# Two feed-forward layers: GpSimd's long subtractions in pieces, early stores moved ahead, one addition moved up

## The reference, cut to what matters

```
g = x @ w_gate;  val = x @ w_val
x = ((g * sigmoid(g)) * val) @ w_out            # first network, hidden width 1536
h = x @ w_in
g = where(h >= 1, h, where(h <= -1, 0, (h + 1)**2 / 4))
out = g @ w_out2                                # second network, hidden width 2048
```

## Time and profile before

| what | value |
|---|---|
| median of 3 runs | 982.42 us (982.23 to 983.0) |
| the profiled execution's own time | 983.68 us |
| its span | 981.9 us |
| TensorE busy | 967.0 us |
| VectorE, ScalarE, GpSimd busy | 704.1, 463.7, 305.1 us |
| chain that ended last: TensorE's share | 86% |

### The profile page before, as it was taken

How to read it: one execution, slowest core, us unless ns; L and a number is a source line. 1 busy time by engine, 2 the same in 40 slices (tenths; PEclk the granted TensorE clock), 3 DMA queues, 4 the chain that set the end, 5 groups by cost and what they waited for, 6 DMA issues and landing times.

```text
span 981.9 us, 18870 instructions
## 1 busy us (share of the span) xinstructions
PE 967.0 (98%) x6372; PEld 926.6 (94%) x6372; DVE 704.1 (72%) x1369; ACT 463.7 (47%) x940; POOL 305.1 (31%) x291
## 2 busy tenths in 40 slices
PE   8999999999999999999999999999999999999998
PEld 7777777999999999999999999999999999999998
DVE  6888989577777555557555568888886777867766
ACT  6899999655445223234222336544543334433331
POOL 5777776166672000100001156575310010000000
PEclk9999999999999999999999999999999999999999
DMA  7554543389878655555555534767775744538321
GB/s 247 166 160 150 170 146 106 122 302 339 321 268 333 244 193 208 223 222 214 217 194 193 207 124 179 251 232 274 277 262 194 286 170 184 208 147 298 138 106 65
DMA packets 46156, 204.72 MB, mean 209 GB/s; under 512 B 5488, under 2 KB 5872, under 8 KB 46064
## 3 DMA queue, kind: packets, MB, share of 16 engines
q1 hardware_dynamic: 45920, 203.52, 56.9%
q10 hardware_dynamic: 144, 0.00, 0.0%
HBM read 147.33 MB, written 56.17 MB: 207 GB/s over the span
## 4 chain that ended last, share of the span: by engine, by line
PE 86%; ACT 5%; issue 3%; DVE 3%; DMA 2%; POOL 1%; SPq 0%; ACTq 0%; DVEq 0%; POOLq 0%
PE ps L1454 25%; PE ps L1455 24%; PE ps L1456 24%; PE ps L1425 5%; PE ps L1368 5%; ACT pt L809 3%; PE ps L1398 3%; DMA kept_ul<-wu_l 1%; DVE xt_l L1109 1%; ACT tmp L919 0%; PE ps L1344 0%; DMA wu_r<-w_up 0%; DVE xy L1224 0%; ACT xt_h L840 0%; DVE negs L1048 0%
## 5 line engine op out<-in xcount | busy, mean ns | idle before, releaser
L1454 PE MATMUL ps<-xt_h,wu_h 128*128 128x384 f32 x840 | 281.4, 335 | 2.7 <-ACT u2s L889 1.7
L1456 PE MATMUL ps<-xt_h,wu_l 128*128 128x384 f32 x840 | 280.8, 334 | 0.0
L1455 PE MATMUL ps<-xt_l,wu_h 128*128 128x384 f32 x840 | 280.8, 334 | 0.0
L1454 PE MATMUL ps<-hid_h,wd_h 128*128 128x384 f32 x672 | 225.5, 336 | 2.9 <-DVE xy L1224 2.4
L1455 PE MATMUL ps<-hid_l,wd_h 128*128 128x384 f32 x672 | 224.6, 334 | 0.0
L1456 PE MATMUL ps<-hid_h,wd_l 128*128 128x384 f32 x672 | 224.6, 334 | 0.0
L1224 DVE TENSOR_TENSOR xy<-xy,ps 128x384 f32<-128x384 f32 x288 | 158.6, 551 | 69.9 <-PE ps L1456 69.1
L904 ACT ACTIVATE hid_h<-hid_r 128x768 fp32r<-128x768 f32 x84 | 70.7, 842 | 201.7 <-DVE hid_r L1198 139.7
L1454 PEld LDWEIGHTS ps<-xt_h,wu_h 128*128 128x128 f32 x840 | 157.7, 188 | 4.6 <-issue 3.5
L1455 PEld LDWEIGHTS ps<-xt_l,wu_h 128*128 128x128 f32 x840 | 157.7, 188 | 0.0
L1456 PEld LDWEIGHTS ps<-xt_h,wu_l 128*128 128x128 f32 x840 | 157.7, 188 | 0.0
(11 more groups left out here) (87 smaller groups left out, 1282.4 us busy)
## 6 DMA issues: line engine op xcount, KB each, us to landing
wu_l<-kept_ul SPq DMA_DIRECT2D x40, 896.0 KB, 7.5
wu_h<-kept_uh SPq DMA_DIRECT2D x40, 896.0 KB, 5.2
kept_uh<-wu_h SPq DMA_DIRECT2D x20, 896.0 KB, 6.8
kept_ul<-wu_l SPq DMA_DIRECT2D x20, 896.0 KB, 8.5
wd_h<-kept_dh SPq DMA_DIRECT2D x28, 512.0 KB, 3.7
wd_l<-kept_dl SPq DMA_DIRECT2D x28, 512.0 KB, 4.7
wu_r<-w_up SPq DMA_DIRECT2D x20, 512.0 KB, 5.1
qk<-qk_in SPq DMA_DIRECT2D x15, 640.0 KB, 4.9
```

The lines of the kernel that those rows point to most:

```text
L1454: nc.tensor.matmul(dst, w_hi, v_hi, start=start, stop=False, skip_group_check=onto)
L1455: nc.tensor.matmul(dst, w_hi, v_lo, start=False, stop=False, skip_group_check=onto)
L1456: return nc.tensor.matmul(dst, w_lo, v_hi, start=False, stop=stop, skip_group_check=onto)
```

## The change

Four edits. **(1)** `up_low` and `down_low` and `x_sum` on GpSimd are issued in pieces: 768 columns as 3 of 256, 512 columns as 2 of 256, and an activation sum of 768 as 2 of 384; the semaphore is raised by the last piece. **(2)** The stores of steps 0 and 1 (three of the four) are issued right after `read_r` of the last pair, ahead of `load_down(0)`; the low part of step 1 follows in step 0. **(3)** In later steps the store of the high part stands ahead of `load_up(u + 2)` and the store of the low part behind it, as before. **(4)** On VectorE, in steps 37 to 43, the first addition `add_down(units[0])` stands ahead of `g_half(u - 1, 1)` instead of behind it.

```diff
-            def keep_up(u):
+            def keep_up_high(u):
                 n = step_index(u)
                 for k in range(3):
                     sp.wait_ge(wu_hi[k], computed_before(u) + 1)
                 sp.dma_start(kept_uh[n].rearrange("p (k n) -> p k n", k=7), wu_h[u % 2][:].bitcast(F32)).then_inc(up_kept_h[u % 2], 16)
+
+            def keep_up_low(u):
+                n = step_index(u)
                 for k in range(3):
                     sp.wait_ge(*low_count(u, k))
                 sp.dma_start(kept_ul[n].rearrange("p (k n) -> p k n", k=7), wu_l[u % 3][:, 1:8].bitcast(F32)).then_inc(up_kept_l[u % 3], 16)
...
             read_r(NPAIR - 1)
+
+            keep_up_high(0)
+            keep_up_low(0)
+            keep_up_high(1)
             for u in range(STEPS):
...
+                if u > 1 and computed(u):
+                    keep_up_high(u)
                 if 0 < u and u + 2 < STEPS:
                     load_up(u + 2)
-                if computed(u):
-                    keep_up(u)
+                if u > 1 and computed(u):
+                    keep_up_low(u)
+                if u == 0:
+                    keep_up_low(1)
...
-                nc.gpsimd.tensor_tensor(wu_l[u % 3][:, a:b], wu_r[u % 3][:, a:b], wu_h[u % 2][:, a - 1:b - 1].bitcast(F32),
-                                        ALU.subtract).then_inc(low_pool[n], 1)
+                for k in range(a, b):
+                    low = nc.gpsimd.tensor_tensor(wu_l[u % 3][:, k], wu_r[u % 3][:, k], wu_h[u % 2][:, k - 1].bitcast(F32),
+                                                  ALU.subtract)
+                low.then_inc(low_pool[n], 1)
...
-                nc.gpsimd.tensor_tensor(wd_l[:, t % 6], wd_r[:, t % 6], wd_h[:, t % 6].bitcast(F32),
-                                        ALU.subtract).then_inc(wd_lo, 1)
+                for a in (0, DM // 2):
+                    cols = slice(a, a + DM // 2)
+                    low = nc.gpsimd.tensor_tensor(wd_l[:, t % 6, cols], wd_r[:, t % 6, cols],
+                                                  wd_h[:, t % 6, cols].bitcast(F32), ALU.subtract)
+                low.then_inc(wd_lo, 1)
...
-                nc.gpsimd.tensor_tensor(raw_sum(sb, n), a, b, ALU.subtract).then_inc(tp, 1)
+                for k in range(2):
+                    part = nc.gpsimd.tensor_tensor(raw_sum(sb, n)[:, k], a[:, k], b[:, k], ALU.subtract)
+                part.then_inc(tp, 1)
...
                 if u > STEPS1:
                     hid_low(tiles_of(u)[0] - 2)
+                    if computed(u):
+                        add_down(units[0])
                     g_half(u - 1, 1)
-                add_down(units[0])
+                if u == STEPS1 or not computed(u):
+                    add_down(units[0])
```

## The result

The changed kernel takes 979.44 us (median of 8 runs, 979.08 to 980.37) where the kernel before takes 982.73 (8 runs): ratio 0.9966, 95% interval 0.9957 to 0.9976, so 2.4 to 4.2 us less. The profiled execution took 979.51 us with a span of 977.7. Forecast were 979.3 and a gain of 3.1.

The account below looks back on a forecast made before the run. TensorE, busy 967.0 of 981.9 us, was taken as the bound. From 983.68 with the profiler, 1.8 for the stores and 1.3 for the second network gave 980.6; the median, 1.26 below, 979.3; range 975.2 to 983.2.

Parts of the forecast that it names:

- The ceiling: TensorE's eight feed-forward waits, 5.4 us listed, each cost about 0.26 more: at most 7.5 us to win.
- The early stores: Around 204 us, stores issued before 184.5 let load_up(3) go earlier and end the u2s wait: 1.8 us gained.
- with sums from 198.9 it just does: Start of step 3: VectorE's up_low(3, 0), after the four sums, ends by 203.5, in time for product 0.
- Pieces in the first network: GpSimd's instructions get longer there by cutting, but TensorE waits for none of this.
- Turns: Second network's step starts: VectorE and GpSimd exclude each other and alternate by instruction; that network gains 1.3 us in sum.
- The walk: Turn-by-turn count of VectorE's chain at step starts: 0.98 us waiting at 41 and 42; 0.58, 0.68 and 0.2 at 38.
- Steps 40 to 42: Start of step 40 loses 0.1 us, starts of 41 and 42 gain 1.4, within step 42 another 0.8.
- The moved addition: VectorE, second network: the first addition ahead of g_half comes early but puts g_half 0.47 us later in the chain.
- (a): Rival: all eight TensorE waits go, 975.4 us; chance 0.20 for a gain of 5 to 8.
- (b): Rival: pieces do nothing on balance or the second network gives back the stores' gain, 982.1 us; 0.25 together with (d).
- (c): Rival: g_half behind the addition lengthens VectorE's chain, needing 1.5 us waiting a start; slower, 986 us; chance 0.10.
- (d): Rival: the early stores do not help, since the load lands late, 981.5 us; chance 0.25 together with (b).

Follow-up runs that it names:

- e9_second_whole: e5_second with GpSimd's down_low of tiles 0, 36 and 37 whole again, one instruction of 512 columns each; 977.04 us, ratio 0.9938 to the kernel before.
- e1_stores: The kernel before with only the store edits 2 and 3, GpSimd's instructions whole and the additions in their old order; 982.42 us, ratio 0.9995.
- e3_move: The kernel before with only edit 4, the first addition moved ahead of g_half; 983.61 us, ratio 1.001.
- e10_early_only: e1_stores with the high part of later steps again stored behind load_up, so edit 2 alone; 982.21 us, 1 run.
- e5_second: The changed kernel with the second addition, add_down(units[1]), also moved ahead of the second hid_low in steps 37 to 43; 977.82 us, ratio 0.9950.
- e4_no_move: The changed kernel with the first addition back in its old place, so edits 1 to 3; 980.38 us, ratio 0.9978 to the kernel before.
- e12_behind: The changed kernel with both additions between g_half and the second hid_low; 982.11 us, ratio 0.9989 to the kernel before.
- e11_order_only: e1_stores with both additions moved ahead and every GpSimd instruction whole, no pieces; 979.01 us, ratio 0.9958 to the kernel before.
- e7_fine: The changed kernel with the weights' low parts in pieces of 128 columns instead of 256; 982.02 us, ratio 0.9989 to the kernel before.

## Why the prediction came out right, point by point

**The ceiling.** That a wait costs 0.26 more than listed, 7.5 us in all, held: e9_second_whole removes all but one of the eight and its span is 6.7 us shorter, 6.4 of it in the feed-forward part; its time is 6.1 less.

**The early stores.** The mechanism was right at each step (stores at 183 to 184, load near 191, first sum at 198.9), the size was not: 1.3 instead of 1.8. A wait at the start of step 3 for `up_low` was one of the prediction's own signs of being wrong, and it came (0.25 listed). The term that failed is "with sums from 198.9 it just does". The four sums took 4.0 us, not 3, because VectorE's operations took turns with them, and VectorE's own `up_low(3, 0)` then waited for a piece. e1_stores shows the same wait longer, with a whole instruction in place of the piece. The 1.8 was also counted from a single execution, whose wait for `u2s` was 1.65; in the unchanged code of e3_move it was 1.06, and from there only 0.6 is gained. By the medians the stores gave 0.4 alone and 1.1 beside the pieces. That edit 3 is worth nothing rests on the one execution of e10_early_only.

**Pieces in the first network** cost TensorE nothing: between product (2, 6) and step 36 the lag changes by 0.1 us in all.

**Turns.** The claim that an instruction of GpSimd stands before each operation of VectorE's chain, and that the sums slip into it, is what the rows at 614 us show: a sum before `s_half` and one before `hid_low`. The starts of 37 and 38 gave back time, at the down that waits for the second addition, as forecast; e5_second, which changes only that addition's place, removes both waits. At step 37 I had 1.1 us lost and it was 0.5. The walk has 0.58 + 0.68 + 0.2 = 1.46 us of turns at step 38, and step 37 "behaves alike". Over an unhindered 0.95, VectorE's three operations wait 0.36 + 0.54 + 0.07 = 0.97 at step 38 and 0.31 + 0.54 + 0.07 = 0.92 at step 37, where `s_half` takes 1.26, `hid_low` 1.49 and `g_half` 1.02. That is 0.2 more than in the kernel before, so with the 0.47 of the moved addition the second one comes 0.7 us later and not 1.1. One of the signs named did not come as stated: the sums began 0.8 us later in their steps, not 0.3 to 0.6 (at 657.79 against 658.37, with a lag of -1.4).

**Steps 40 to 42.** Here the walk was too dark. It had 0.98 us of turns before the second addition, the rows show 0.57, and the half microsecond of slack holds it but for 0.05. So the forecast waits at 41 and 42 did not come, and step 40 gained 0.6 instead of losing 0.1. This is 1.1 us in the trace, and with the 0.6 of step 37 it outweighs the 0.5 of the stores: the trace is 1.3 us better than the sum. The median is 3.3 us lower and the span 4.2, because the profiled execution of the kernel before was 0.9 us slower than its median; 0.6 of that is the longer wait at 204 us. The other profiled executions began the feed-forward part 0.3 us earlier to 0.7 later than that one. That 979.44 lies so close to the forecast of 979.3 is luck in part: the stores gave less and the second network more than forecast, and both sizes were counted from one execution.

**The moved addition.** I priced it as a cost of 0.47 in the chain. e3_move bears that out at steps 37 and 38, which are 0.2 and 0.6 us longer there. e4_no_move shows its other side, which the prediction did not work out: where an activation sum delays `g_half`, an addition behind it is late too. e12_behind says so most plainly.

**The rivals.** (a), all waits gone, was not this kernel; e9_second_whole comes near it. (b), nothing on balance, fell: the gain is 2.4 to 4.2 us. The chain of (c) is what e3_move shows by itself, for a loss of 0 to 0.2%; the stall of 1.5 us a start that (c) needs did not come, the rows have 0.92 and 0.97. (d), the load lands late, fell: it lands early enough for a first sum at 198.86.

## What to carry to other kernels

Where two engines exclude each other, cutting the long instruction helps the one that would wait for it and costs the one that is cut: more time of its own and a turn lost at each cut. Keep whole what another engine is about to need: `down_low` of the next group, whole in e9_second_whole. That cutting pays elsewhere is shown by e9_second_whole against e11_order_only, for all the other pieces together; no run cuts the activation sums alone against the same order uncut. Look first at what stands behind a wait in an engine's queue: moving a short addition into 0.9 us of idle time gave 1.6 us, and with both additions ahead the changed kernel's time was reached with no piece at all. And compare the profiled execution with the median before a size is read from it: here one was 0.9 us off, and in e4_no_move 1.1.

## What the runs showed of the hardware

Between two engines that both read two tiles of SBUF, a queued stream of short GpSimd instructions does not keep VectorE out: in the rows at 614 and 661 us VectorE gets in after at most one of them, and GpSimd after one of VectorE's. The two `down_low` of step 37, 1024 columns, took 2.53 us as two instructions (e9_second_whole; 2.99 in the kernel before), 3.27 and 4.26 as four (changed kernel, e5_second), 4.88 as eight (e7_fine), with what VectorE took in between. Who pays beside `x_sum` hangs on a few tenths. Before, `s_half` is recorded at 662.59 and `x_sum` at 662.60, and `s_half` lost 1.7 us; in e3_move `x_sum` started 0.37 us behind `s_half`, and `hid_low` after it lost 1.2. In the first pair the one recorded 10 ns earlier is the one that waited, so recorded starts this close do not tell which was first. The wait for `u2s` at 204 us was 1.65 us before and 1.06 in e3_move, whose code up to there is the same: `load_up(3)` went out at 195.11 instead of 195.88 and the first sum started at 199.48 instead of 200.34.
